# Another order for the first steps of a fused attention, expert and dense kernel

## The reference

```python
# attention with a decaying state: batch 4, 8 heads, 768 tokens, head size 48
state = np.zeros((B, H, D, D))
for t in range(S):
    kt, vt, rt = k[:, :, t], v[:, :, t], r[:, :, t]
    cur = np.einsum('bhd,bhe->bhde', u[None] * kt, vt)
    y[:, :, t] = np.einsum('bhd,bhde->bhe', rt, state + cur)
    state = w[None, :, :, None] * state + np.einsum('bhd,bhe->bhde', kt, vt)
# x: y as 3072 rows of 384
# experts: each row goes to the one of 8 experts with the largest logit
logits = x @ w_gate
expert_idx = np.argmax(logits, axis=1)
h = np.maximum(xe @ w1[e], 0.0)       # 384 -> 1024, for the rows xe of expert e
out[mask] = gate_w[mask, None] * (h @ w2[e])
# dense: 384 -> 2048 -> 384
h = x @ w_in
return np.maximum(0.01 * h, h) @ w_out
```

## Time and profile before

| what | us |
|---|---|
| median of 3 runs | 826.67 (822.53 to 831.79) |
| the profiled execution | 826.78 |
| its span, first to last instruction | 825.0 |
| TensorE busy in it | 777.6 |
| VectorE busy | 335.7 |
| GpSimd busy | 335.2 |
| ScalarE busy | 215.4 |

### The profile page before, as it was taken

One profiled execution on the slowest core, in us unless ns is written; L12 is line 12 of the kernel. 1 busy time (PEld: TensorE's weight loads), 2 busy tenths in 40 slices (PEclk: granted clock), 3 DMA queues, 4 the chain that ended last, 5 costly groups with the idle time before them and its releaser, 6 DMA issues.

```text
span 825.0 us, 17781 instructions
## 1 busy us (share of the span) xinstructions
PE 777.6 (94%) x7216; PEld 714.8 (87%) x7216; DVE 335.7 (41%) x659; ACT 215.4 (26%) x436; POOL 335.2 (41%) x337
## 2 busy tenths in 40 slices
PE   9888889929999999999899999999999999999995
PEld 8777778729999999999889989989988998998994
DVE  8667565442332233223555333433433433433332
ACT  1234332411221121212132232232232223222221
POOL 6477775426679787977991010010010001001001
PEclk9699887959999999999999999999999999999998
DMA  5666665145653555455440010010000000001001
GB/s 145 184 190 173 178 180 177 59 141 114 129 158 106 136 154 151 108 133 149 110 122 9 1 39 0 1 39 1 1 38 0 0 0 38 0 0 39 1 1 39
DMA packets 42611, 66.91 MB, mean 81 GB/s; under 512 B 11413, under 2 KB 31797, under 8 KB 42549
## 3 DMA queue, kind: packets, MB, share of 16 engines
q1 hardware_dynamic: 28944, 50.76, 22.0%
q10 hardware_dynamic: 10533, 5.80, 3.7%
q0 software_dynamic: 3072, 9.45, 3.1%
HBM read 51.42 MB, written 14.59 MB: 80 GB/s over the span
## 4 chain that ended last, share of the span: by engine, by line
PE 92%; DVE 3%; issue 2%; DMA 1%; POOL 0%; ACTq 0%; ACT 0%; DVEq 0%; POOLq 0%
PE bank L1159 24%; PE bank L1138 24%; PE bank L1083 13%; PE bank L1099 12%; PE ps_y L818 4%; PE ps_y L803 2%; PE ps_x L775 2%; PE ps_s L755 2%; PE ps_x L771 2%; PE ps_l L839 1%; PE ps_x L830 1%; PE ps_s L853 1%; PE ps_m L789 1%; PE bank L1066 1%; DMA rows<-x_rows 1%
## 5 line engine op out<-in xcount | busy, mean ns | idle before, releaser
L1027 POOL DMA_INDIRECT out_rows<-rows,ids_i x24 | 23.1, 962 | 358.7 <-ACT rows L1238 353.2
L1303 DVE TENSOR_TENSOR h_lo<-gf,h_hi 128x512 fp32r<-128x512 f32 x96 | 71.7, 747 | 225.7 <-ACT h_hi L1229 225.7
L134 POOL TENSOR_TENSOR w_lo<-stage,w_hi 128x768 fp32r<-128x768 f32 (+1 forms) x70 | 146.1, 2087 | 5.8
L1159 PE MATMUL bank<-w_hi,h_hi 128*128 128x384 f32 x384 | 130.4, 340 | 1.1 <-DVE h_lo L1303 1.1
L1159 PE MATMUL bank<-w_lo,h_hi 128*128 128x384 f32 x384 | 129.3, 337 | 0.0
L1159 PE MATMUL bank<-w_hi,h_lo 128*128 128x384 f32 x384 | 129.1, 336 | 0.0
L1225 ACT ACTIVATE hc<-bank 128x512 f32<-128x512 f32 x96 | 57.4, 598 | 272.0 <-PE bank L1138 272.0
L1138 PE MATMUL bank<-x_hi,w_hi 128*128 128x512 f32 x288 | 113.4, 394 | 2.4 <-DVE x_lo L1285 2.3
L1138 PE MATMUL bank<-x_lo,w_hi 128*128 128x512 f32 x288 | 113.6, 395 | 0.0
L1138 PE MATMUL bank<-x_hi,w_lo 128*128 128x512 f32 x288 | 113.4, 394 | 0.0
L1266 DVE SCALAR_TENSOR_TENSOR h_lo<-bank,h_hi 128x416 fp32r<-128x416 f32 x64 | 37.8, 591 | 142.0 <-ACT h_hi L1205 142.0
(11 more groups left out here) (166 smaller groups left out, 1202.5 us busy)
## 6 DMA issues: line engine op xcount, KB each, us to landing
stage<-in_moe_w SPq DMA_DIRECT2D x24, 512.0 KB, 6.1
stage<-in_moe_w SPq DMA_DIRECT2D x32, 384.0 KB, 3.1
rows<-x_rows ACTq DMA_DIRECT2D x9, 625.6 KB
x_rows<-pad_row SPq DMA_DIRECT2D x32, 156.4 KB
k_u<-in_k SPq DMA_DIRECT2D x48, 96.0 KB, 2.5
r_u<-in_r SPq DMA_DIRECT2D x48, 96.0 KB, 2.9
v_u<-in_v SPq DMA_DIRECT2D x24, 192.0 KB, 3.4
stage<-in_moe_w_in SPq DMA_DIRECT2D x6, 512.0 KB, 4.1
```

Of the source, the lines that this page charges most:

```text
L134: i = eng.tensor_tensor(w_lo[:, buf, off:off + cols], stage[:, h, 0:cols], w_hi[:, buf, off:off + cols].bitcast(F32), ALU.subtract)
L1159: i = pe.matmul(ps_o[t][:, 0:D], x[:, f % NB, t * P:(t + 1) * P], ww[:, 1, o:o + D], start=f == 0 and x is h_hi and ww is w_hi, stop=f == ...
L1303: dve.tensor_tensor(h_lo[:, f % NB, :], gf[:, f % 2, :], h_hi[:, f % NB, :].bitcast(F32), ALU.subtract).then_inc(gl_ok, 1)
```

## The change

The instructions are the same but for eight filler products fewer. What changes is their place. On VectorE one memset of `r_u` (buffer 0) is gone to GpSimd; `ps_m` is cleared behind the powers, `x_st` behind the scaling of unit 1, which itself now stands behind the masks of unit 0; the six conversions of the tables stand in step 3. On GpSimd the buffers 3 and 4 are cleared behind the mask, `pad_row` and `wg` in step 0, the integer tables in step 1. SP waits for the first transfer of unit 0 on one memset instead of two, loads `k` before `r`, and waits for GpSimd's memset between them. The new helper `due(g)` names the units scaled in step g, on both engines: g + 2 in steps 0 to 3, units 6 and 7 in step 4, and g + 3 from step 5 on.

```diff
--- before.py
+++ after.py
@@ -274,7 +274,7 @@
             route = sem("route")
             RS = 16
             AHEAD = 3
-            WARM = 36
+            WARM = 28
             OWN = 2
 
 
@@ -293,6 +293,13 @@
 
             def slot(c, j):
                 return (2 * c + j) % 4
+
+            def due(g):
+
+
+
+                last = min(g + 2 if g < HP else g + AHEAD, UN - 1)
+                return range(g + 2 if g <= HP else g + AHEAD, last + 1)
 
             def routed(c, q):
 
@@ -319,6 +326,9 @@
                     (c, q), i = divmod(g, HP), g % RB
                     for t in range(2):
                         sp.dma_start(k_u[heads[t], i, :, :], k[c, q, t]).then_inc(rk_in[i], 16)
+                    if g == 0:
+                        sp.wait_ge(rows_pool, 1)
+                    for t in range(2):
                         sp.dma_start(r_u[heads[t], i, :, :], r[c, q, t]).then_inc(rk_in[i], 16)
                     sp.dma_start(v_u[:, i, 0:B * W2].rearrange("p (t b d) -> p t b d", t=2, b=B),
                                  v[c, q]).then_inc(v_in[i], 16)
@@ -331,9 +341,9 @@
 
 
                     if g < OWN:
-                        sp.wait_ge(rows_dve, 2 * g + 2)
+                        sp.wait_ge(rows_dve, 2 * g + 1)
                     else:
-                        sp.wait_ge(rows_pool, 2 * (g - OWN) + 2)
+                        sp.wait_ge(rows_pool, 2 * (g - OWN) + 3)
                     if g == 0:
                         sp.wait_ge(zeros_ok, 1)
                     load(g)
@@ -365,10 +375,10 @@
 
                 pool.memset(ones[:, :], 1.0).then_inc(warm_ok, 1)
                 pool.wait_ge(warm_ok, 1)
-                for i in range(OWN, RB):
-                    for a in (k_u, r_u):
-                        pool.memset(a[DH // 32 * 32:L, i, :, :], 0.0).then_inc(rows_pool, 1)
-                pool.wait_ge(rows_pool, 2 * (RB - OWN))
+                pool.memset(r_u[DH // 32 * 32:L, 0, :, :], 0.0).then_inc(rows_pool, 1)
+                for a in (k_u, r_u):
+                    pool.memset(a[DH // 32 * 32:L, OWN, :, :], 0.0).then_inc(rows_pool, 1)
+                pool.wait_ge(rows_pool, 3)
                 pool.memset(ident[:, :], 0.0).then_inc(tables, 1)
                 pool.wait_ge(tables, 1)
                 pool.affine_select(out=ident[:, :], in_=ident[:, :], compare_op=ALU.not_equal, fill=1.0,
@@ -381,6 +391,10 @@
                 for j in range(2):
                     pool.tensor_copy(mask_l[halves[j], :], mask[halves[j], halves[j]]).then_inc(consts, 1)
                     pool.wait_ge(consts, j + 2)
+                for i in range(OWN + 1, RB):
+                    for a in (k_u, r_u):
+                        pool.memset(a[DH // 32 * 32:L, i, :, :], 0.0).then_inc(rows_pool, 1)
+                pool.wait_ge(rows_pool, 2 * (RB - OWN) + 1)
 
                 def scaled_k(g):
                     (c, q), i = divmod(g, HP), g % RB
@@ -421,25 +435,27 @@
                                        ALU.add, ALU.add).then_inc(ids_ok1, 1)
 
                 pc = expert_pieces(0)
-                pool.memset(tick[:, :], 0.0).then_inc(tables, 1)
-                pool.iota(slot_no[:, :], [[1, LOOKS]], base=0, channel_multiplier=0).then_inc(tables, 1)
-                pool.iota(rank_no[:, :], [[-1, E]], base=E, channel_multiplier=0).then_inc(tables, 1)
-                pool.iota(region_no[:, :], [[RR, E]], base=U, channel_multiplier=0).then_inc(tables, 1)
-                pool.iota(limit_no[:, :], [[U, MORE]], base=U, channel_multiplier=0).then_inc(tables, 1)
-                pool.iota(tok_no[:, :, :], [[P, YB], [S, B]], base=0, channel_multiplier=1).then_inc(tables, 1)
                 pool.wait_ge(small, 16 * 2)
                 pool.wait_ge(powers, 1)
-                for g in range(AHEAD):
+                for g in range(2):
                     scaled_k(g)
-                pool.memset(pad_row[:, :], 0.0).then_inc(zero_ok, 1)
-                pool.memset(wg[:, :, :], 0.0).then_inc(zero_ok, 1)
                 own_terms(0)
                 for g in range(UN):
                     c, q = divmod(g, HP)
-                    if g + AHEAD < UN:
-                        scaled_k(g + AHEAD)
+                    for n in due(g):
+                        scaled_k(n)
                     if g + 1 < UN:
                         own_terms(g + 1)
+                    if g == 0:
+                        pool.memset(pad_row[:, :], 0.0).then_inc(zero_ok, 1)
+                        pool.memset(wg[:, :, :], 0.0).then_inc(zero_ok, 1)
+                    if g == 1:
+                        pool.memset(tick[:, :], 0.0).then_inc(tables, 1)
+                        pool.iota(slot_no[:, :], [[1, LOOKS]], base=0, channel_multiplier=0).then_inc(tables, 1)
+                        pool.iota(rank_no[:, :], [[-1, E]], base=E, channel_multiplier=0).then_inc(tables, 1)
+                        pool.iota(region_no[:, :], [[RR, E]], base=U, channel_multiplier=0).then_inc(tables, 1)
+                        pool.iota(limit_no[:, :], [[U, MORE]], base=U, channel_multiplier=0).then_inc(tables, 1)
+                        pool.iota(tok_no[:, :, :], [[P, YB], [S, B]], base=0, channel_multiplier=1).then_inc(tables, 1)
                     if c >= YB and q == 0:
                         token_numbers(c)
                     if c >= 2 and q in STORE_AT:
@@ -462,16 +478,13 @@
                     dve.wait_ge(chain_v, steps[0])
 
                 dve.memset(wu_col[:, :, :], 1.0).then_inc(cleared, 1)
+                dve.memset(k_u[DH // 32 * 32:L, 0, :, :], 0.0).then_inc(rows_dve, 1)
                 dve.memset(v_u[:, :, B * W2:], 0.0).then_inc(zeros_ok, 1)
-                for i in range(OWN):
-                    for a in (k_u, r_u):
-                        dve.memset(a[DH // 32 * 32:L, i, :, :], 0.0).then_inc(rows_dve, 1)
+                for a in (k_u, r_u):
+                    dve.memset(a[DH // 32 * 32:L, 1, :, :], 0.0).then_inc(rows_dve, 1)
                 dve.sem_inc(route, RS)
                 dve.memset(pw[:, :, :, T0:T0 + 1], 1.0)
-                dve.memset(ps_m[:, :, 0:B * DH], 0.0)
                 dve.memset(v_st[:, :, :], 0.0)
-                dve.memset(x_st[:, :, 0, :], 0.0)
-                dve.memset(x_st[:, :, 1:, B * DH:], 0.0)
 
                 dve.wait_ge(small, 16 * 2)
                 link(dve.reciprocal(wu_col[:, 1, :], wu_col[:, 1, :]))
@@ -589,17 +602,13 @@
                             ins = dve.tensor_copy(row_i[:, i3, :], keep[:, 0, :])
                         ins.then_inc(route, 1)
 
-                for g in range(2):
-                    scale(g)
+                dve.memset(ps_m[:, :, 0:B * DH], 0.0)
+                scale(0)
                 dve.wait_ge(consts, 3)
                 masks(0)
-                dve.wait_ge(tables, 7)
-                dve.tensor_copy(rank[:, :], rank_no[:, :])
-                dve.tensor_copy(region[:, :], region_no[:, :])
-                dve.tensor_copy(run[:, 0, :], region_no[:, :])
-                dve.tensor_copy(limit[:, :], limit_no[:, :])
-                dve.tensor_copy(yc[:, :, :, D:D + 1], tok_no[:, :, :].unsqueeze(3))
-                link(dve.tensor_copy(slot_n[:, :], slot_no[:, :]))
+                scale(1)
+                dve.memset(x_st[:, :, 0, :], 0.0)
+                dve.memset(x_st[:, :, 1:, B * DH:], 0.0)
                 for g in range(UN):
                     c, q = divmod(g, HP)
                     if g > 0:
@@ -610,10 +619,16 @@
                     if c < C - 1:
                         state(g, 1)
                     routing(routed(c, q))
-                    if g == 0:
-                        scale(2)
-                    if g + AHEAD < UN:
-                        scale(g + AHEAD)
+                    for n in due(g):
+                        scale(n)
+                    if g == 3:
+                        dve.wait_ge(tables, 7)
+                        dve.tensor_copy(rank[:, :], rank_no[:, :])
+                        dve.tensor_copy(region[:, :], region_no[:, :])
+                        dve.tensor_copy(run[:, 0, :], region_no[:, :])
+                        dve.tensor_copy(limit[:, :], limit_no[:, :])
+                        dve.tensor_copy(yc[:, :, :, D:D + 1], tok_no[:, :, :].unsqueeze(3))
+                        link(dve.tensor_copy(slot_n[:, :], slot_no[:, :]))
                 rows_out(UN - 1)
 
                 dve.wait_ge(last_mm, 1)
```

## The result

The changed kernel takes 817.76 us (median of 20 runs, 810.84 to 825.59) against 825.37 (815.78 to 833.17): ratio 0.9915, 95% interval 0.9892 to 0.9939, or 7.0 us less (5.0 to 8.9). Two later comparisons of the same kernel gave 0.9922 (0.9882 to 0.9962) and 0.9923 (0.9888 to 0.9959).

What follows compares the result with a forecast made beforehand. TensorE, busy 94% of the span, was taken as the bound, losing time to early waits and low clock. Unit 6 9.5 us sooner, less 2.3 of stalls, gave 7.2: 826.8 to 819.6, range 814 to 826.

Steps and rivals of the forecast that it cites:

- (1) to (3): Start on VectorE, SP and GpSimd: scaling 0 about 1.5 us earlier, scores of unit 0 at 9.35 against 11.06.
- (4), (5): Scaling 1 and steps 0 to 3: unit 1 scores at 13.2, steps of 4.25 us, unit 6 at 35.7 before stalls.
- (6): Tables and small work in steps 0 to 3: six VectorE conversions cost 0.64 to 3.8 us, taken as 0.
- (7): TensorE stalls named "issue" before unit 6: not removed by the diff, taken as 1.16 us twice.
- The sum: Gain at unit 6 of 9.5 us less 2.3 of stalls: 7.2, giving 819.6 from 826.8.
- Everything after shifts as a block: After unit 6: unchanged work of a nearly always busy TensorE, so the gain reaches the end whole.
- A: Rival, early steps: the clock falls all the same after a stall, costing 2.73 us, 822.3; chance 0.20.
- B: Rival, before unit 6: no stall in the new stretch, 817.3; chance 0.18.
- C: Rival, step 4: the pile-up only moves to the scalings of units 6 and 7, 824.3; chance 0.12.
- D: Rival, from unit 1 on: gaps and less filler leave TensorE at 1.2 GHz, slower at 832.8; chance 0.05.
- E: Rival, loads: unit 0 lands after 6.9 or unit 5 after 27, 821 to 822; chance 0.05.

Runs made afterwards that it cites:

- e1: Kernel before with only one scaling in each of the first four steps, scaling 1 behind unit 0's masks; ratio to before 1.0014 (0.9959 to 1.0069).
- e2: Kernel before with only the new start: moved memsets, split loads of unit 0, 28 filler products; ratio to before 1.003 (0.9971 to 1.009).
- e3: Changed kernel with step 3's six table conversions moved between state and masks; ratio to before 1.0013 (0.9967 to 1.0059).
- e8: Changed kernel with conversions between state and masks and first expert weights issued in steps 2 and 3; ratio to before 0.9926 (0.9889 to 0.9964).
- e10: Changed kernel with the first two pieces of expert weights issued in steps 2 and 3, a repeat run; ratio to before 0.9935 (0.9899 to 0.9972).
- e7: Changed kernel with a lead of two units to the end, no doubled scaling in step 4; ratio to before 0.9958 (0.9918 to 0.9997).
- e9: The kernel before, unchanged, run again for a second trace; ratio to before 0.9987 (0.9956 to 1.0019).
- e12: The changed kernel, unaltered, run a third time; ratio to before 0.9923.
- e11: Kernel of e10 with 92 filler products instead of 28, delaying the first layer; ratio to before 1.0111 (1.0073 to 1.0148).
- e5: The changed kernel, unaltered, run again on another chip; ratio to before 0.9922 (0.9882 to 0.9962).
- e4: Changed kernel with 36 filler products again instead of 28; ratio to before 1.0115 (1.0056 to 1.0174).

## Why the prediction held

Forecast 819.6 from 826.8, a gain of 7.2; measured 7.0, and 817.76 by the median. That the doubled scaling and the late start held TensorE up, and that what is saved there reaches the end, held. That the two gains agree to 0.2 us is luck: unit 6 did not come as early as forecast, one term was wrong in kind, and more was gained behind unit 6 than in the sum, which put nothing there.

**(1) to (3), the start.** Scaling 0 at 6.94 (forecast 6.9), the `k_u` product over at 9.29 (9.3), SP's loads in time. Where I had TensorE stand 0.5 for it, the filler was still running: 56 records took 8.53, not 7.8, since the first of them are slower than the mean (9 records between 1 and 3 us, 28 between 7 and 9.6, in the first trace of the changed kernel). Scores of unit 0 at 9.57 instead of 9.35. The powers and the filler are now nearly tied.

**(4), (5), the loop.** Scores of unit 1 at 13.64 (13.2); next steps 4.21 and 4.39 (4.25). TensorE stood 0.17, 0.36 and 0.16 before the scores of units 2 to 4, less than the 0.4 of the forecast. e1 gives the same pace with the old start. That the doubled scaling causes the wait of 2 us is shown by e2, where it stays, and by e1, where it goes.

**(6), the conversions.** I took 0 of a range 0.64 to 3.8. They took 2.26, and held up the rows of unit 3, the state of unit 4 and through it ScalarE's copy, for which TensorE stood 0.84. This term was wrong in kind: the low row I leaned on had met the end of one GpSimd product, here they met two. e3 shows that the conversions are short in the other place, e8 against e10 that TensorE's wait goes with them. This wait and a long stall in the scores of unit 4 do not add: where the stall was 1.55 or more, the wait was not there.

**(7), the stalls.** Two of 1.16 forecast, 2.3; before unit 6 the trace has 0.34, 1.00 and 0.53, 1.87. In other executions the one at 602 alone was 1.55 twice and 2.10 (e3, e7).

**The sum.** Unit 6 at 39.12 instead of 38.0: 0.84 from the conversions, about 0.75 from start and steps, less 0.45 of stalls. 6.06 us were gained there in the first pair of traces, 5.3 in the second (e9 and e12). The 7.0 at the end is 1 to 2 more, and its interval (5.0 to 8.9) holds both. By the first expert product the lead had grown to 8.9 and 7.2 us, with less time at the low clock before it: 30 us against 53 in the first pair, 26 against 36 in the second. The forecast had no term for that; how much of it is the change and how much chance, no run shows. "Everything after shifts as a block" holds for the middle of many runs (e11) and not for a pair of traces.

**The rivals.** A, the fall of the clock before unit 6, was there in e5 and e12 and not in the first trace, so forecast and A are both parts of one kernel's spread rather than alternatives; the price of 2.73 was for a longer stretch than the 3.4 us of e12. B did not happen: none of the three traces of the changed kernel was without stalls. C did not happen: in none of the three does TensorE wait for `x_st` in step 5, and e7 gained nothing by taking the doubling out. D did not happen in any trace: gaps of 0.36 before the scores brought no fall. E did not either: no scaling up to unit 5 waited for its load in the first trace. How the 7 us divide between the start and the scalings in time was not settled: e1 and e2 ran on the chip whose times tell nothing at this size. In the first pair of traces 1.5 of the 6.06 at unit 6 were there at unit 0.

## What to carry to other kernels

Look in the trace for two scalings, or any two long products with two SBUF inputs, one behind the other on VectorE while GpSimd has its own: the second waits for GpSimd's queue, and what stands behind it comes late. Small work put behind such a product pays the same wait; put it where the engine waits for another anyway (2.26 us in the one place, 0.76 in the other). Where a gap has no named cause, add up the engine's own products ahead of it in two kernels, and look when the packets of its instruction queue come in. Judge an edit at the start of a long kernel by the milestone right behind it and by many runs, not by one pair of ends.

## What was not expected of the hardware

TensorE's gaps named issue lie for the most part at fixed counts of its own products, 475, 602, 855 and so on, whatever the work there. They last from 0.3 to 2.4 us, and in the first traces of both kernels they end 1.2 to 1.6 us after a packet of its own instructions has come in. In the five traces of the two kernels (before, changed, e5, e9, e12) the clock fell 16 times in the first 150 us. 14 of these falls began during or within 2 us behind such a gap, of 1.2 to 2.2 us, and the other two at the wait of 2 us for the state; other gaps of that size brought none (1.34 us before 58.77, changed kernel).

Filler products are no fixed time: 72 records took 10.02 us in one trace and 10.98 in e4. They run at two paces, 0.21 us a record at first and 0.11 later, and the later pace set in at 4.8 us in the one and 7.0 in the other, while the rows give the clock as 1.00 all along. Of the three traces of the changed kernel it set in at 5.4, 5.8 and 6.2, and the scores of unit 0 start at 9.50, 9.65 and 9.90 in their timelines: part of what a single trace shows at the start is this chance. 64 more products cost 13.8 us, 0.215 each. One chip ran the same kernel 2% slower by the median of all runs (843.88 against 823 to 828 us).
